# Attention and two expert layers on one core: kv loaded in stripes, scatters in halves, and the end of the program laid out twice

## The reference

```python
kv_pool = kv.reshape(B, H // 4, 4, W // 4, 4, C).mean(axis=(2, 4))   # kv: 2 x 384 x 32 x 128
kv_flat = kv_pool.reshape(B, -1, C) @ w_sr                            # 768 keys a batch; k = v
a = softmax(q @ k.T / sqrt(C));  x = a @ v
# layer 1: each token goes to the one expert of the largest logit
e = argmax(x @ w_gate);  x = gate_w * (relu(x @ w1[e]) @ w2[e])
# layer 2: the same with other weights, and a sigmoid output gate
e = argmax(x @ w_gate2); out = gate_w * sigmoid(x @ w_output_gate)[e] * (relu(x @ w1b[e]) @ w2b[e])
```

## Time and profile before

| | us |
|---|---|
| median of 3 runs | 1969.69 (1968.4 to 1975.17) |
| the profiled execution | 1974.21 |
| its span, first to last instruction | 1972.5 |
| PE busy | 1906.3 (97%) |
| DVE busy | 1325.6 (67%) |
| ACT busy | 1078.4 (55%) |
| POOL busy | 743.9 (38%) |

### The profile page before, as it was taken

The page is one execution under the profiler, slowest core; times in us unless marked ns, Lnnn a source line. Parts: engine busy times, 40 slices in busy tenths (PEclk is TensorE's granted clock), DMA queues, the critical chain, the costliest instruction groups (busy, mean ns, idle before and its releaser), DMA issues.

```text
span 1972.5 us, 53309 instructions
## 1 busy us (share of the span) xinstructions
PE 1906.3 (97%) x15870; PEld 1885.2 (96%) x15870; DVE 1325.6 (67%) x3505; ACT 1078.4 (55%) x2333; POOL 743.9 (38%) x821
## 2 busy tenths in 40 slices
PE   4799999999999899999999999999999999999998
PEld 3799999999999899999999999989999999999998
DVE  6577887777778576666666666756655555555554
ACT  2577777777777544444444444434454444444543
POOL 4456663366663232233223223323333333333333
PEclk9899999999999999999999999999999999999999
DMA  9355542145541321111241111141211114241111
GB/s 244 87 174 179 179 158 71 58 154 172 181 168 68 128 75 49 49 52 53 69 150 49 52 49 52 54 171 43 70 44 43 43 43 168 64 140 46 44 43 32
DMA packets 141496, 185.89 MB, mean 94 GB/s; under 512 B 17809, under 2 KB 95764, under 8 KB 137824
## 3 DMA queue, kind: packets, MB, share of 16 engines
q1 hardware_dynamic: 116096, 134.16, 22.5%
q0 software_dynamic: 25312, 50.65, 7.3%
HBM read 98.41 MB, written 87.63 MB: 94 GB/s over the span
## 4 chain that ended last, share of the span: by engine, by line
PE 92%; DMA 3%; SPq 2%; issue 1%; DVE 1%; POOL 0%; ACT 0%; POOLq 0%; DVEq 0%; ACTq 0%
PE psum L1203 28%; PE psum L1220 28%; PE psum L1119 10%; PE psum L1079 10%; PE psum L1103 6%; PE psum L1235 2%; PE psum L1138 2%; PE psum L1187 2%; SPq L658 1%; PE psum L1066 1%; PE psum L1237 1%; DMA w_split<-w_table 1%; DMA y_bucket<-kv_store,place 1%; DMA kv_store<-in_kv 1%; DMA q_in<-in_q 1%
## 5 line engine op out<-in xcount | busy, mean ns | idle before, releaser
L1614 DVE SCALAR_TENSOR_TENSOR h_lo<-psum,h_hi 128x512 fp32r<-128x512 f32 x800 | 553.0, 691 | 413.6 <-ACT h_hi L1410 411.5
L1410 ACT ACTIVATE h_hi<-psum 128x512 fp32r<-128x512 f32 x800 | 478.6, 598 | 638.2 <-PE psum L1203 635.3
L1203 PE MATMUL psum<-x_hi,w 128*128 128x256 f32 x1600 | 375.7, 297 | 5.4 <-issue 3.0
L390 POOL DMA_INDIRECT y_bucket<-kv_store,place x200 | 195.9, 979 | 474.5 <-DVE place L362 425.7
L1203 PE MATMUL psum<-x_hi,w_split 128*128 128x256 f32 x1600 | 365.6, 291 | 7.8 <-DMA w_split<-w_table 3.9
L1220 PE MATMUL psum<-h_hi,w 128*128 128x256 f32 x1600 | 354.4, 284 | 1.7 <-DVE h_lo L1614 1.7
L951 POOL DMA_INDIRECT out<-rows x200 | 194.6, 973 | 407.1 <-DVE rows L1634 369.3
L390 POOL DMA_INDIRECT x_bucket<-rows,place x192 | 189.7, 988 | 310.2 <-DVE place L362 264.3
L1203 PEld LDWEIGHTS psum<-x_hi,w 128*128 128x128 f32 x1600 | 277.8, 191 | 6.2 <-issue 5.2
L1203 PEld LDWEIGHTS psum<-x_hi,w_split 128*128 128x128 f32 x1600 | 273.5, 189 | 9.0 <-issue 9.0
L1220 PEld LDWEIGHTS psum<-h_hi,w 128*128 128x128 f32 x1600 | 279.0, 192 | 2.2 <-DVE h_lo L1614 2.2
(11 more groups left out here) (174 smaller groups left out, 4190.7 us busy)
## 6 DMA issues: line engine op xcount, KB each, us to landing
w_table<-w_split SPq DMA_DIRECT2D x64, 512.0 KB, 3.8
w_raw<-in_moe_w SPq DMA_DIRECT2D x64, 256.0 KB, 4.6
xr<-x_bucket SPq DMA_DIRECT2D x100, 132.0 KB, 2.5
xr<-y_bucket SPq DMA_DIRECT2D x100, 132.0 KB, 2.6
kv_store<-in_kv SPq DMA_DIRECT2D x48, 256.0 KB, 12.2
q_in<-in_q SPq DMA_DIRECT2D x48, 256.0 KB, 2.8
w<-w_table SPq DMA_DIRECT2D x12, 1024.0 KB, 5.3
w_split<-w_table SPq DMA_DIRECT2D x8, 1024.0 KB, 6.6
```

The lines of the kernel that those rows point to most:

```text
L390: nc.gpsimd.indirect_dma_start(r.bucket[:, :], bass.IndirectOffsetOnAxis(r.place[:, g, s:s + 1], 0), r.rows[:, g, s, LG:], None, bounds_ch ...
L1203: ins = nc.tensor.matmul(bank[p][:, m * BLOCK:(m + 1) * BLOCK], layer.w1[c % 2][:, hl, f], x[:, c % 2, :], start=k == 0, stop=k == 2)
L1410: nc.scalar.activation(h_hi[:, p, :], bank[p][:, :], ACT.Relu).then_inc(h_hi_done, 1)
L1614: nc.vector.scalar_tensor_tensor(h_lo[:, p, :], bank[p][:, :], 0.0, h_hi[:, p, :].bitcast(F32), ALU.max, ALU.subtract).then_inc(h_lo_done, 1)
```

## The change

- **kv in stripes.** A stripe is 32 rows of the image, contiguous in HBM: one DMA of 512 KB, 128 partitions with 4 KB each (two windows of 4 pixels of one image row). There are 12 stripes in a batch. DVE (batch 0) and POOL (batch 1) add in two steps, 2 x 256 and 2 x 128 elements a partition, over the 4 pixels of a window; what is left of the pooling, over the four image rows, is a sum over partitions, and PE does it together with the transpose: four matmuls a chunk against `key_of`, a 128 x 32 matrix of ones and zeros.
- **Order of the lead.** Query groups 0, 1 and 2 are loaded after stripe 5 of batch 0, after the last one, and after stripe 3 of batch 1. PE, ACT and DVE turn the first two query blocks between the chunks, and PE scores block 0 against the first half of the keys before the last chunk. Batch 1's stripes wait for PE's step (`kv_turned`) and no longer for DVE's sum.
- **Scatters in halves.** A group's four indirect DMAs become two and two, with a semaphore for each half. The first half goes when the places are done, the second when PE has made the second turn of the next block (attention) or the second up step of the next tile (layer 1); for the last two groups of the attention it is the second up step of layer 1's tiles 1 and 3. In between POOL does one of the two weight splits. Who writes a slot waits for its own half alone.
- **The tests.** The test is `If_eq(last, 0)`: the case of 100 tiles comes right behind it, and the other behind that. Layer 2 is a function that is written out in both cases, for PE, ACT and DVE. SP and POOL keep their tests.
- DVE's write of tile 99's rows no longer waits for the scatter by itself; `skipped` waits for it at its start.

```diff
@@ load_kv, SP
-                    if b:
-                        sp.wait_ge(kv_summed, c + 1)
-                    for k in range(POOL):
-                        sp.dma_start(kv_in[:, c, k, :], src[k]).then_inc(kv_loaded[c], 16)
+                    if b:
+                        sp.wait_ge(kv_turned, k // 2 + 1)
+                    sp.dma_start(kv_in[:, k].rearrange("p a j c -> p (a j c)"),
+                                 kv[b, k * STRIPE:(k + 1) * STRIPE].rearrange("h (w r) c -> (h w) (r c)", r=RUN)) \
+                        .then_inc(kv_loaded[k], 16)
+                for k in range(STRIPES):
+                    load_kv(0, k)
+                    if k == 1:
+                        sp.dma_start(wsr[:, :], w_sr).then_inc(wsr_in, 16)
+                    if k == 5:
+                        load_q(0, 0)
+                load_q(0, 1)
...
+                for k in range(STRIPES):
+                    load_kv(1, k)
+                    if k == 3:
+                        load_q(0, 2)
@@ scatter
-                wait(pool, r.place_done, i, 2, gc + 1)
+                if h == 0:
+                    wait(pool, r.place_done, i, 2, gc + 1)
+                elif r.n == 1 and live(i, 2 * gc + 5, NBLK, UNROLL):
+                    wait(pool, p_turned, i, PAIRS * UNROLL, PAIRS * (2 * gc + 5) + 2)
+                else:
+                    wait(pool, up_done, i - NIT if r.n == 1 else i, HP * UNROLL, HP * (2 * gc + 5) + 2)
                 pool.sem_inc(r.scatter_go, 1)
-                for s in range(GSUB):
+                for s in range(h * SUB, (h + 1) * SUB):
@@ POOL, an iteration of the attention
                         group(i, gc)
                         if item is not None:
                             split(n, item, 2 * gc)
+                        scatter(pool, r1, i, gc, 1)
+                        if item is not None:
                             split(n, item, 2 * gc + 1)
@@ tiles
-                with eng.If_ne(eng.to_reg(last), 0):
+                with eng.If_eq(eng.to_reg(last), 0):
+                    body(TIT - 2, 1)
+                    skipped()
+                    second_layer(eng, body)
+                with eng.Else():
                     body(TIT - 2, 1)
                     body(TIT - 1, 1)
-                with eng.Else():
-                    body(TIT - 2, 1)
-                    skipped()
+                    second_layer(eng, body)
@@ PE
+                def pool_keys(n, ps):
+                    for k in (2 * n, 2 * n + 1):
+                        for a in range(2):
+                            at = ((k % 2) * 2 + a) * (P // 4)
+                            ins = nc.tensor.matmul(ps[:, at:at + P // 4], kv_in[:, k, a, 0, :],
+                                                   key_of[:, :, :].rearrange("p h w -> p (h w)"), start=True, stop=True)
+                    ins.then_inc(kv_turned, 1)
...
                 def lead():
-                    turn_q(0, 0)
-                    turn_q(0, 1)
+                    pe.wait_ge(key_of_done, 1)
+                    for n in range(KC):
+                        pe.wait_ge(kv_summed, 2 * n + 2)
...
+                        pool_keys(n, first_keys(n))
...
+                        project(n, first_kv(n))
+                        if n == 2:
+                            pe.wait_ge(const_pool, 3)
+                            turn_q(0, 0)
+                        if n == 3:
+                            turn_q(0, 1)
+                        if n == KC - 2:
+                            pe.wait_ge(kv_lo_done, KC // 2)
+                            for s in range(SUB):
+                                score(0, 0, s, 0, (0,))
                     pe.wait_ge(kv_lo_done, KC)
                     pe.wait_ge(const_in, 48)
-                    score(0, 0, 0, 0)
-                    score(0, 0, 1, 0)
+                    for s in range(SUB):
+                        score(0, 0, s, 0, (1,))
@@ rows_out (ACT); tile_rows_out (DVE) is changed in the same way
-                        wait(act, r1.scattered[g], i, 64, 64 * (c // 4))
+                        wait(act, r1.scattered[g][c % 2], i, 32, 32 * (c // 4))
@@ kv_sum (DVE); POOL's folds are the same two steps
-                    nc.vector.tensor_reduce(pooled[:, n % 2, :], kv_in[:, n].rearrange("p i (j c) -> p c (i j)", c=C),
-                                            AX.X, ALU.add).then_inc(kv_summed, 1)
+                    for k in (2 * n, 2 * n + 1):
+                        dve.wait_ge(kv_loaded[k], 16)
+                        nc.vector.tensor_tensor(kv_in[:, k, :, 0:2, :], kv_in[:, k, :, 0:2, :], kv_in[:, k, :, 2:4, :],
+                                                ALU.add).then_inc(kv_halved, 1)
+                        dve.wait_ge(kv_halved, k + 1)
+                        nc.vector.tensor_tensor(kv_in[:, k, :, 0, :], kv_in[:, k, :, 0, :], kv_in[:, k, :, 1, :],
+                                                ALU.add).then_inc(kv_summed, 1)
@@ skipped (DVE)
+                    dve.wait_ge(r2.scattered[1][1], 32 * (TIT - 2))
```

More of the change, by code:

```diff
@@ L79, in moe_kernel @@
     KC = NKEY // P
+    RUN = 2 * POOL
+    STRIPE = P * RUN // WW
+    STRIPES = HH // STRIPE
     PAIRS = KC // 2
@@ L575, in moe_kernel @@
         const_pool = sem("const_pool")
+        ident_done = sem("ident_done")
+        key_of_done = sem("key_of_done")
         const_dve = sem("const_dve")
[L577 removed]
+        kv_loaded = [sem(f"kv_loaded{k}") for k in range(STRIPES)]
+        kv_halved = sem("kv_halved")
         kv_summed = sem("kv_summed")
@@ L696, in iteration @@
                     for h in range(2):
-                        if live(i, 2 + h, NGRP, 2):
+                        if live(i, 2 + h, NGRP, 2) and not (isinstance(i, int) and i == h == 0):
                             load_q(i, 2 + h)
@@ L772, in early @@
                     for g in range(2):
-                        sp.wait_ge(plan.r.scattered[g], 64 * EARLY_GROUPS // 2)
+                        for h in range(2):
+                            sp.wait_ge(plan.r.scattered[g][h], 32 * EARLY_GROUPS // 2)
                 def body(i, n):
@@ L872, in _ @@
                                    neutral[:, :, :]).then_inc(neutral_out, 16)
[L874 to L884, removed]
+                for k in range(STRIPES):
+                    pool.wait_ge(kv_loaded[k], 32)
+                    pool.tensor_tensor(kv_in[:, k, :, 0:2, :], kv_in[:, k, :, 0:2, :], kv_in[:, k, :, 2:4, :],
+                                       ALU.add).then_inc(kv_fold, 1)
+                    pool.wait_ge(kv_fold, FOLDS * k + 1)
+                    pool.tensor_tensor(kv_in[:, k, :, 0, :], kv_in[:, k, :, 0, :], kv_in[:, k, :, 1, :],
+                                       ALU.add).then_inc(kv_fold, 1)
                 def group(i, gc):
-                    wait(pool, r1.scattered[gc], i, 64, 0)
+                    for h in range(2):
+                        wait(pool, r1.scattered[gc][h], i, 32, 0)
                     rid = rows[:, gc % 2, :, LG + ID].bitcast(I32)
@@ L928, in _ @@
                     for gc in range(2):
-                        scatter(pool, r2, i, gc)
+                        for h in range(2):
+                            scatter(pool, r2, i, gc, h)
                 last = layers[1].last(pool, plan1)
@@ L1004, in tiles @@
                     body(i, 2)
-                with eng.If_ne(eng.to_reg(last), 0):
-                    body(LAST_BODY - 2, 2)
-                    body(LAST_BODY - 1, 2)
-                    body(LAST_BODY, 2)
-                with eng.Else():
+                with eng.If_eq(eng.to_reg(last), 0):
                     limit[0] = 2 * TILES - UNROLL
@@ L1013, in tiles @@
                     limit[0] = 2 * TILES
+                with eng.Else():
+                    body(LAST_BODY - 2, 2)
+                    body(LAST_BODY - 1, 2)
+                    body(LAST_BODY, 2)
             limit = [2 * TILES]
@@ L1068, in turn_q, with score @@
                     ins.then_inc(q_turned, 1)
-                def score(i, c, s, batch):
+                def score(i, c, s, batch, halves=(0, 1)):
                     if not live(i, c, NBLK, UNROLL):
@@ L1075, in score @@
                     wait(pe, probs_done, i, 2 * UNROLL, 2 * (c - 1) + s + 1)
-                    for m in range(2):
+                    for m in halves:
                         keys = slice(batch * KC + m * (KC // 2), batch * KC + (m + 1) * (KC // 2))
@@ L1376, in lead @@
                 def lead():
-                    q_high(0, 0)
-                    q_high(0, 1)
+                    for n in range(KC):
+                        kv_scale(n, first_keys(n))
+                        kv_high(n, first_kv(n))
+                        if n in (2, 3):
+                            q_high(0, n - 2)
                     exps(0, 0, 0)
@@ L1526, in lead @@
                 def lead():
-                    q_low(0, 0)
-                    q_low(0, 1)
+                    kv_sum(0)
+                    for n in range(KC):
```

(5 more changed lines are left out.)

126 lines of the change are left out of this document (59 added, 67 removed).

## The result

The changed kernel takes 1938.69 us (median of 4 runs, 1937.46 to 1940.45), against 1972.37 of the kernel before beside it (4 runs, 1968.4 to 1975.17): ratio 0.9831, interval 0.9808 to 0.9855. That is 1.7% faster, and clear of the noise. The prediction was 1930 in a range of 1923 to 1945. The profiled execution took 1937.6 us with a span of 1935.9, 36.6 less than the span before (the forecast's sum was 39.7).

What follows compares the result with a forecast made beforehand. PE was taken as the bound, with its idle and low-clock time to be won: 23.2 (lead and stall) + 9.9 (scatters) + 6.6 (tests) = 39.7 off 1974.2, less the 4.5 offset, gives 1930 us, range 1923 to 1945.

Steps and rivals of the forecast that it cites:

- The stall: PE's 11.5 us wait for query group 2 goes, with 1.7 us of low clock behind it: 13.2 us.
- The halves: Scatter waits at the attention's end, 996 us and 1301 us shrink, as readers wait for two DMAs only: 9.9 us.
- The tests: At the two tile-count tests PE falls through, so waits of 2.27 and 2.58 us and 1.7 of clock go: 6.6 us.
- POOL ends last anyway: At the program's end, the jumps out of the cases stand behind each engine's last work and cost nothing.
- The sum: Whole kernel: 23.2 for lead and stall, 9.9 for scatters, 6.6 for tests, together 39.7 us off the profiled 1974.2.
- the lead: Start of the kernel up to steady attention blocks: faster kv loads and shorter key sums make it 10.0 us shorter.
- the offset: Whole time: the profiled execution lies 4.5 us above the median of the runs, and the same is taken after.
- the rate stays: Rival, chance 0.2: kv loads in the lead stay at 252 GB/s in stripes, gain 12 for 23.2, 1941 us.
- halves don't help: Rival, chance 0.1: the first half of a scatter lands behind the weights as well, 1940 us.
- the tests still fetch: Rival, chance 0.1: the code behind each tile-count test is new to PE either way, 1937 us.
- the second half is late: Slower rival, chance 0.04: ACT or DVE waits for a scatter's second half in all 98 groups, 2028 us at 1 us each.
- up to 1.1 us a stripe for POOL's folds beside DVE's additions: Lead, last one to three stripes: by the shared-interface rule up to 1.1 us each more, lead 1 to 3 us longer.

Runs made afterwards that it cites:

- order: Kernel before with only the third query group's load moved, to behind the second chunk of batch 1: 1960.45 us, ratio 0.9939.
- contig: Kernel before with each kv load taken from one contiguous 256 KB piece, 2 KB descriptors kept, other keys summed: ratio 0.993, in a disturbed set.
- halves_again: Kernel before with the scatters in halves alone, second and undisturbed run: 1957.93 us, ratio 0.9944.
- stripes: Kernel before with kv in stripes, new lead and earlier third query group, scatters and tests as before: ratio 0.9941, in a disturbed set.
- tests_again: Kernel before with only the order of the cases behind the tile-count tests changed, second run: 1966.58 us, ratio 0.9974.

## Why the prediction was right, and where it was off

**The stall**: 11.5 + 1.7 = 13.2 was forecast, and from block 0 to layer 1 the time is 13.2 less (622.2 to 609.0), but by two errors that cancel. The key matmuls of the six late chunks take 0.97 where a transpose took 0.27: 6 x 0.7 = 4.2, which I had left out. It can be followed: from block 0 to the last late chunk's wait `order` takes 79.4 us and the changed kernel 83.3. Against it, each group of two blocks took 0.09 less, as below. My reason for the stall, the place in the queue, is shown by `order`; by `contig` the higher rate alone takes the wait away as well.

**The halves**: 9.9 forecast, 11.3 in layer 1 alone. I had counted half of the 3.2 us of low clock behind 672 us; all of it went. The reason, that the reader waits for the first two of four scatters, is shown by `halves_again`. But in `stripes` PE's wait at the end of the attention was gone with whole scatters. So what the halves are worth inside the changed kernel, among its 15.3 us in layer 1, is not shown by itself; it is taken from the run of them alone. That the waits of 1.6 for den_g and of 1.3 before layer 2 would stay was right.

**The tests**: 6.6 forecast, 4.6 in the trace and 5.1 in the runs of the edit alone. Both fetches go, as I said. By the Trainium skill's rule on taken branches ("Runtime: NRT & Kernel Launch", "Instruction fetch mechanics") a jump out of what was fetched ahead waits for a fetch, and the traces agree, with a block of 16 KB loaded at each wait behind such a jump. What failed is "POOL ends last anyway": the tail is 6.5 to 7.5 in all eight kernels that hold layer 2 twice, and 5.6 or 5.7 in the six that hold it once, though POOL's last scatters come in the same rhythm. In the last 9 us the eight load 6 to 8 instruction blocks, the six at most one; in the changed kernel the first comes at once when PE has ended. So the jumps out of the cases do bring fetches, and I had put them at nothing. That the end waits for them is likely, but no run shows it.

**The sum**: 39.7 against 36.6: the lead 2.6 less, the layers 0.5 more, the tail 1.0 less. That 36.6 comes so near to 39.7 is in part luck, as errors of 4.2 and 3.9 us cancel in the stall. The other 5.6 of the 8.7 us between 1930 and 1938.7 are the offset: I took 4.5 off the profiled time because three runs had a median of 1969.69, and the profiled time after is 1.1 below its median. In two later sets the kernel before had medians of 1972.0 (6 runs) and 1971.6 (14).

**The rivals**: "the rate stays" fell with 404 GB/s, "halves don't help" with `halves_again`, "the tests still fetch" with `tests_again`, and the second half is late nowhere: but for the 1.2 us before layer 2, PE waits behind no scatter in the list above. What I gave as up to 1.1 us a stripe for POOL's folds beside DVE's additions was 1.5 (1.75 + 0.84 for 0.69 + 0.42) on the last stripe alone, and none of it was on the path.

## What to carry to other kernels

Ask of a wait for data first where the transfer stands in its queue: one load's place was a third of this gain, and the rate, which looked like the cause, wasn't needed for it, though it would have done as well. Count small fp32 matmuls by the records of the same type and clock, and price them, and all that follows up to the first steady block, at the low clock where PE has gaps. A jump at the end of a program is a jump too. And weigh a median of three runs as little as one profile when the sum is set against it.

## What the runs showed of the hardware

- Loads of kv that step by 64 KB between 2 KB pieces ran at 251 GB/s from 12 to 22 us in one trace and at 267 to 297 in five others; the same pieces from one contiguous range at 387, 4 KB pieces at 402 to 405.
- What PE did in its waits told on the clock: with transposes in them the first key matmuls still took 1.92 us, with bf16 matmuls 1.08. The clock then fell behind a wait of 1.48 us in one kernel (0.50 from 16 to 32 us), and stayed up through the lead where that was filled. Up to its first rise the granted clock reads 1.00 even where durations are those of 0.50 (0.63 us for a turn at both, 0.38 at the high level).
- A jump to a case that isn't next cost PE 2.3 to 2.8 us in six places and 6.05 in one, with one instruction block of 16 KB loaded at each of the six waits and two at the seventh.
- A DVE addition of 128x512 elements with both inputs in SBUF took 0.68 us alone and 1.75 beside a POOL addition of the same form.
- In all four undisturbed kernels with stripes a group of two attention blocks takes 12.57 us, and 12.66 in all four without, though the loop has the same instructions; single fp32r matmuls are 1 to 2 ns shorter in the means (337 to 335). Over the attention that is 3.9 us. The code and tiles around differ, but which of them does it stays open. The starts of one group and the next, before and after:
```profile
317.16 0.19 PE L277 MATMUL psum<-onehot,before 128*128 128x32 bf16 x1
329.82 0.19 PE L277 MATMUL psum<-onehot,before 128*128 128x32 bf16 x1
```
```profile
299.19 0.19 PE L279 MATMUL psum<-onehot,before 128*128 128x32 bf16 x1
311.75 0.19 PE L279 MATMUL psum<-onehot,before 128*128 128x32 bf16 x1
```
